# RWKV attention and two MoE layers on one core: blank matmuls left out of the attention's loop over groups

## The reference, cut to what matters

```python
# attention: B, H, S, D = 2, 8, 768, 48
for t in range(S):
    cur = einsum('bhd,bhe->bhde', u[None] * kt, vt)
    y[:, :, t] = einsum('bhd,bhde->bhe', rt, state + cur)
    state = wt[:, :, :, None] * state + einsum('bhd,bhe->bhde', kt, vt)
x = attn_out.transpose(0, 2, 1, 3).reshape(B * S, H * D)          # 1536 x 384
# two MoE layers: 8 experts, top-1, hidden size 1024
logits = x @ w_gate (+ modality_bias[modality_id] in the first)
out[mask] = gate_w[mask, None] * (relu(x[mask] @ w1[e]) @ w2[e])
```

## Time and profile before

| | us |
|---|---|
| median of 3 runs | 589.34 (588.6 to 589.96) |
| span of the profiled execution | 583.4 |
| TensorE busy | 510.3 (87%) |
| VectorE busy | 417.1 (71%) |
| ScalarE busy | 350.5 (60%) |
| GpSimd busy | 147.9 (25%) |

### The profile page before, as it was taken

How to read it: one execution, slowest core, us unless ns; L and a number is a source line. 1 busy time by engine, 2 the same in 40 slices (tenths; PEclk the granted TensorE clock), 3 DMA queues, 4 the chain that set the end, 5 groups by cost and what they waited for, 6 DMA issues and landing times.

```text
span 583.4 us, 10333 instructions
## 1 busy us (share of the span) xinstructions
PE 510.3 (87%) x3044; PEld 421.6 (72%) x3044; DVE 417.1 (71%) x745; ACT 350.5 (60%) x517; POOL 147.9 (25%) x127
## 2 busy tenths in 40 slices
PE   5389889898999769999988999936999999999993
PEld 2267777676877448898866888823888888888982
DVE  1484887788574667888766888536788889888881
ACT  3235335524422147888767888503697998889881
POOL 4141343234043020332222324200213222212121
PEclk9697999999599788999999999969899999999997
DMA  9606368457410725010766110035777776401000
GB/s 148 78 2 169 76 175 189 145 109 164 135 36 0 256 65 194 28 41 24 239 237 228 34 41 24 28 118 151 262 268 240 266 263 237 154 23 34 23 27 4
DMA packets 85760, 71.99 MB, mean 123 GB/s; under 512 B 57796, under 2 KB 77342, under 8 KB 85744
## 3 DMA queue, kind: packets, MB, share of 16 engines
q1 hardware_dynamic: 80096, 62.20, 37.7%
q0 software_dynamic: 4096, 9.55, 4.9%
q10 hardware_dynamic: 1552, 0.05, 0.1%
HBM read 66.64 MB, written 8.31 MB: 128 GB/s over the span
## 4 chain that ended last, share of the span: by engine, by line
PE 49%; issue 19%; DMA 14%; DVE 7%; POOL 5%; ACT 2%; DVEq 1%; POOLq 1%; ACTq 0%; SPq 0%
PE bank L919 12%; PE bank L885 11%; DMA xrow<-x_rows,gidx 6%; PE bank L924 6%; PE bank L896 5%; PE bank L903 4%; DMA x_rows<-yrow,sidx 3%; DVE K L979 2%; PE bank L681 2%; POOL rk L437 2%; DMA out_dram<-yrow,sidx 2%; PE bank L780 2%; DMA w1s<-in_moe_w_dram 1%; PE bank L858 1%; DMA w2s<-in_moe_w_dram 1%
## 5 line engine op out<-in xcount | busy, mean ns | idle before, releaser
L1219 DVE TENSOR_TENSOR w_parts<-w1s,w_parts 128x1536 fp32r<-128x1536 f32 x60 | 105.3, 1758 | 31.5 <-ACT w_parts L609 30.6
L1227 DVE TENSOR_TENSOR w_parts<-w2s,w_parts 128x768 fp32r<-128x768 f32 x120 | 108.4, 956 | 3.6 <-ACT w_parts L616 3.6
L885 PE MATMUL bank<-w_parts,xT_hi 128*128 128x512 f32 x360 | 101.2, 412 | 2.2 <-ACT xT_hi L623 2.2
L609 ACT ACTIVATE w_parts<-w1s 128x1536 fp32r x60 | 88.6, 1479 | 21.5 <-SPq L354 12.6
L681 PE MATMUL bank<-blank 128*128 128x512 bf16 (+3 forms) x268 | 78.5, 364 | 23.6 <-DVE T L993 9.1
L919 PE MATMUL bank<-w_parts,hT_hi 128*128 128x384 f32 x480 | 97.3, 344 | 0.4
L616 ACT ACTIVATE w_parts<-w2s 128x768 fp32r x120 | 94.5, 836 | 4.9 <-PE bank L924 2.4
L919 PEld LDWEIGHTS bank<-w_parts,hT_hi 128*128 128x128 f32 x480 | 83.4, 188 | 6.1 <-issue 6.0
L474 POOL DMA_INDIRECT xrow<-x_rows,gidx x34 | 43.8, 1289 | 161.7 <-issue 91.7
L885 PEld LDWEIGHTS bank<-w_parts,xT_hi 128*128 128x128 f32 x360 | 69.2, 197 | 16.2 <-issue 1.9
L681 PEld LDWEIGHTS bank<-blank 128*128 128x128 bf16 x268 | 34.4, 134 | 46.6 <-issue 22.0
(11 more groups left out here) (153 smaller groups left out, 754.8 us busy)
## 6 DMA issues: line engine op xcount, KB each, us to landing
w1s<-in_moe_w_dram SPq DMA_DIRECT2D x16, 1536.0 KB, 6.8
w2s<-in_moe_w_dram SPq DMA_DIRECT2D x16, 1536.0 KB, 7.3
raw_w<-in_w_dram SPq DMA_DIRECT2D x16, 144.0 KB, 7.2
raw_r<-in_r_dram SPq DMA_DIRECT2D x16, 144.0 KB, 4.6
raw_k<-in_k_dram SPq DMA_DIRECT2D x16, 144.0 KB, 4.2
v<-in_v_dram SPq DMA_DIRECT2D x8, 288.0 KB, 3.1
x_rows<-out_pair SPq DMA_DIRECT2D x4, 576.0 KB, 8.6
xrow<-x_rows,gidx POOLq DMA_INDIRECT x34, 3.6
```

The costliest lines, as they stand in the source:

```text
L609: nc.scalar.activation(w1c[:, HI, :, cols], w1s[:, bass.ds(s, 1), :, cols].rearrange("p a k n -> p (a k) n"), ACT.Copy).then_inc(w1_hi[m], 1)
L885: nc.tensor.matmul(h_ps[f][:], xT[HI][:, q, :], w1c[:, z, q, cols], start=(q == 0 and z == HI), stop=False)
L1219: nc.vector.tensor_tensor(w1c[:, LO, :, cols], w1s[:, bass.ds(s, 1), :, cols].rearrange("p a k n -> p (a k) n"), w1c[:, HI, :, cols].bitca ...
L1227: nc.vector.tensor_tensor(w2c[:, LO, ks, :].rearrange("p k n -> p (k n)"), w2s[:, bass.ds(s, 1), ks, :].rearrange("p a k n -> p (a k n)"), ...
```

## The change

In the loop over groups, all calls of `keep_warm` go: one behind every second `coefficient`, ten in the last group, one before every second `logits`, two before each half's wait for the states, one before each chunk of output products, and one before each chunk of scores. That is 22 in each group and 10 more in the last, 186 in all. Those of the prologue (`first`) and of the routing stay. Nothing else is changed.

```diff
@@ body
                 def small(c):
                     coefficient(g, par, c)
-                    if c % 2:
-                        keep_warm(lg_ps[:])
@@
                     for c in range(CH):
                         small(c)
-
-                    for _ in range(10):
-                        keep_warm(lg_ps[:])
@@
                 scores(g, par, 0)
                 for c in range(CH):
-                    if c % 2:
-                        keep_warm(lg_ps[:, CH * E:])
                     logits(g, c, evacuated)
@@
                     pe.wait_ge(yy_evac, 2 * g + 1 + f)
-                    for _ in range(2):
-                        keep_warm(yy_ps[f][:])
                     pe.wait_ge(state_ready, g + 1)
                     pe.wait_ge(sc_masked, 2 * g + f + 1)
                     for c in range(CF * f, CF * f + CF):
-                        keep_warm(yy_ps[f][:, CF * HD:])
@@ scores
                 for c in range(CF * f, CF * f + CF):
-                    keep_warm(sc_ps[0][:, CF * P:])
                     for hh in range(2):
```

## The result

The changed kernel takes 623.95 us (median of 4 runs, 620.75 to 624.48), the kernel before 589.65 us in the same comparison: a ratio of 1.058, 95% interval 1.054 to 1.061. It is slower by 34.3 us; 620 us had been predicted, with a range of 599 to 624.

The account below looks back on a forecast made before the run. No engine bounds the loop throughout; TensorE is on the path for output products. With the clock staying down, +25.4 us to the seventh group, +4.9 last group and +1.1 tail add +31.4 to 589.34: 620.7, stated 620, range 599 to 624.

Parts of the forecast that it names:

- the wait that would have been three times as long: TensorE's wait for the states in a warm group, ahead of the output products: from 1.09 to about 3.5 us.
- the prediction's two reasons: Why the clock stays down: falls follow waits for the states, which lengthen; rises followed raw transposes with blanks, now removed.
- T to `rk`: Lower clock, from T (second half of a group's output in `out_pair`) to GpSimd's `rk`: 7.85 us.
- step 2: Scores, logits and chunk sums at the lower clock, TensorE the bound: 6.8 us, bounds 6.0 to 7.1; warm 3.53.
- step 3: C and the states on VectorE, not slower: 0.2 us to C, then 2.93 us, reaching 18.2 us.
- step 4: Output products at the lower clock: first chunk 0.78 us, five others of 1.18, 6.68 us in all.
- step 5: From the last output product to the next T: 0.6 us, making a cold group 25.4 us.
- The first group: States ready as before at 40.16 us, output at 47.5 against 48.26 us: -0.8 us.
- The six groups to the seventh T: Six cold groups of 25.4 us, T at 199.9 against 174.47 us: +25.4 with the first group's -0.8 included.
- The last one: Last group, without raw transposes, at the lower clock: 22.7 against 17.8 us, +4.9 us.
- The clock comes back in each group: Rival: clock rises among raw transposes, falls at each wait for the states; 22.8 us a group, 601 us, chance 0.25.
- The clock holds: Rival: clock falls at two places as now, blanks a pure cost of 1.02 us a group; 581 us, chance 0.07.

Follow-up runs that it names:

- e4: Kernel before with all 186 loop blanks left in place but each only 8 columns wide; 630.38 us, ratio 1.068.
- e3: Changed kernel plus twelve blanks of 512 columns ahead of the first half's wait for the states, none elsewhere in the loop; 599.24 us, ratio 1.014.
- e5: Kernel before with seven blanks of 512 columns instead of two ahead of the first half's wait for the states; 578.08 us, ratio 0.986.
- e6: Kernel before with seven blanks instead of two at the first half's wait and none on the path of the output products; 568.18 us, ratio 0.972.
- e1: Kernel before without the 8 blanks a group on the path of the output products, the other 14 kept; 600.59 us, ratio 1.015.
- e7: Changed kernel plus twelve blanks ahead of the first half's wait and three among the raw transposes of each group; 581.31 us, ratio 0.994.
- e8: Changed kernel plus only the three blanks among the raw transposes of each group; 609.45 us, ratio 1.041.
- e2: Kernel before with only the 8 blanks a group on the path of the output products kept, the off-path ones removed; 635.01 us, ratio 1.076.

## Why the prediction was right, and where its steps were off
The direction and the cause hold. Without the blanks TensorE runs at its lower clock through the loop, and with that it becomes the bound of the part ahead of the states. e4 separates the clock from the instructions, and e3, e5 and e6 show that blanks at the wait for the states bring the clock back or keep it, and the time with it.

Where the clock is lost was right for the kernel before and for e1, and not for the changed kernel. Its three falls in the loop, at 30.7, 81.9 and 160.4 us, came at the last raw transposes of a group or just behind them, while the first scores began at 32.27, 84.00 and 161.50 us. So the clock never reached a wait for the states at its full level, and the wait that would have been three times as long had no part in it. Of the prediction's two reasons the second, that the raw transposes lose their blanks, is the one that fits; e7 against e3 bears it out.

Step by step, for the group from 101.52 us on:
- *T to `rk`*: 7.92 us against 7.85; the last `K128` transpose ends at 8.51 against 8.25.
- *Scores, logits, sums* (step 2): 6.53 us against 6.8, inside the bounds. The sum was near by luck, because two errors met: scores take 1.59 us, not 2.4, and logits and sums 4.94 instead of 4.4. The warm times had been read from stretches with blanks: 1.26 us for the scores, where e3 shows 0.87 without them, and 1.1 and 1.17 us for logits and sums, where e3 shows 1.36 and 1.26.
- *C and states* (step 3): C 15.14 us after T (15.05 + 0.2); the output products 3.01 us later (2.93). TensorE still waits 1.47 us there, where I had said that it hardly waits: the scores of the second half are short too.
- *Output products* (step 4): from 119.67 us to the next T (127.55) are 7.88 us; less the 0.63 from the last product to T (step 5) that is 7.25, against 6.68. The term was taken from a stretch with narrow blanks (1.18 us a chunk); without them a chunk takes 1.28. Where the narrow blanks stood they cost 0.18 us and took 0.10 from the product behind them.
- Group: 26.0 us against 25.4.

The sum of differences inside the span was +31.4 us and should have been +39.3. The first group gave +1.5 instead of -0.8 (T at 49.80 us, 48.26 before), since the clock fell at 30.7 us, behind the raw transposes, and not at the wait: its first output product came at 41.92 us, where 40.16 had been taken over from before. The six groups to the seventh T (205.48 against 174.47 us) bring it to +31.0, instead of +25.4. The last one took 23.15 us (+5.3; +4.9 predicted). Routing began 37.9 us later than before (236.48 against 198.56 us), 1.6 us more than the end of attention (1.1 predicted), and 1.4 us more came in the MoE stages, for which nothing had been put.

That 620 still lay within 4 us of the median, and the median 0.05 us inside the range, is partly luck in the base. The span of the kernel changed is 1.8 us below its own execution's time, that of the kernel before 5.9 below the median of its runs; if 1.8 us also lie around that span, its execution took some 585.2 us, 4 us less than the median to which I added the difference. So the estimate of the difference was 8 us too small and the base 4 too high.

*The rivals.* "The clock comes back in each group" is wrong for the change: it came back twice, for 3 us. It is the pattern of e1, where a group takes 23.9 us. By the Trainium skill's rule on sustained activity (TensorE: Matmul & The Clock Gate, "The HAM clock gate") it should have come back. The traces disagree: here TensorE was busy 93% of 75 us at clock 0.50, and in e4 97% of 149.5 us. "The clock holds", with its price of 581 us, was seen only with more blanks at the wait: e6 is that case. Its price was built on 1.02 us a group; 0.65 is measured.

What stays open is how the places combine. With seven or twelve blanks at the wait no fall comes there, and it comes at the next place that has none: the raw transposes (e3), scores, logits and sums (e7), and in e6, which has blanks in both, nowhere before the end of attention. But e5 has blanks everywhere and still falls once, in the chunk sums, and e1 (the wait as before, no blanks in the output products) loses the clock where the kernel before mostly keeps it. Nor is the place separated from the mere amount: the clock in the loop mostly rises with the third column too. Against amount alone stand e8 over e2 (3 wide blanks' worth against 4.6) and e6 over e7 (14.2 against 15); no run moves the same blanks from one place to another.

## What to carry to other kernels
Filler matmuls are to be judged by the granted clock from end to end of the loop, not by their own time: 22 of them a group cost 0.65 us on the path at full clock and were worth 5 or 6. Here they did best when most of their work stood in the matrix engine's wait for another engine, as many as end just when the wait does (seven; two, seven and twelve were tried), and with these in place the ones between products on the path could go. Cover the other thin stretches too: a place left without blanks is where the clock was lost next in e3 and e7.

## What the runs showed of the hardware that was not expected
- Of the four-byte products, those of 48 rows and 128 columns (the scores) grow least at the lower clock: 0.87 to 1.59 us for six, a factor of 1.83; output products go from 0.67 us a chunk to 1.28 without blanks, 1.91. Three raw transposes grow less than either, from about 0.38 us (e3: 49.37 to 49.74, 50.11 to 50.50) to 0.67 (changed kernel: 103.30 to 103.97), 1.76.
- A narrow blank between products is partly hidden: at the lower clock the chunk is 1.36 us with it (0.18 + 1.18) and 1.28 without, while the three among the scores of a half cost more than their own length: 1.74 us with them (75.93 to 77.67 us in the trace of before) against 0.87.
- The clock can fall without any idle time of TensorE: in e5 none is printed from 69.69 us to the fall at 75.8 us, and blanks of 128 to 512 columns stood among the transposes, scores and logits of that stretch.
